# A fused attention and two-MLP kernel: order of value products, loads, one weight tile and the last product

## The reference

```python
scores = cap * tanh((q @ k.T / sqrt(64)) / cap)
attn = exp(scores - max(scores)); attn = attn / (sum(attn) + 1e-9)
x = (attn @ v), heads side by side                    # 896 x 768
x = relu(x @ w_in1) ** 2 @ w_out1                     # 768 x 2048, 2048 x 768
x = silu(x @ w_in2) @ w_out2                          # 896 x 768
```

## Time and profile before

| | |
|---|---|
| median of 3 executions | 543.65 us (543.34 to 544.69) |
| profiled execution | 543.38 us, span 541.6 us |
| TensorE (PE) busy | 530.9 us, 98% |
| VectorE (DVE) | 361.9 us, 67% |
| ScalarE (ACT) | 261.0 us, 48% |
| GpSimd (POOL) | 80.0 us, 15% |
| granted clock of TensorE | 0.998 mean |

### The profile page before, as it was taken

The page is one execution under the profiler, slowest core; times in us unless marked ns, Lnnn a source line. Parts: engine busy times, 40 slices in busy tenths (PEclk is TensorE's granted clock), DMA queues, the critical chain, the costliest instruction groups (busy, mean ns, idle before and its releaser), DMA issues.

```text
span 541.6 us, 7075 instructions
## 1 busy us (share of the span) xinstructions
PE 530.9 (98%) x2616; PEld 439.8 (81%) x2616; DVE 361.9 (67%) x623; ACT 261.0 (48%) x404; POOL 80.0 (15%) x54
## 2 busy tenths in 40 slices
PE   7999999999999999999999999999999999999996
PEld 5233334799999999999998999999999999999995
DVE  3298787687678634667789835556855345568985
ACT  5999995155443333444444344444433144454230
POOL 1899999100000000000000000000000000000000
PEclk9999999999999999999999999999999999999999
DMA  8789601051202202422022024211210241020546
GB/s 225 203 229 222 188 15 31 29 154 42 79 0 79 58 2 60 136 58 78 0 79 60 0 59 136 59 41 37 71 50 16 59 136 41 19 79 10 120 65 89
DMA packets 82117, 42.17 MB, mean 78 GB/s; under 512 B 26784, under 2 KB 79008, under 8 KB 82080
## 3 DMA queue, kind: packets, MB, share of 16 engines
q1 hardware_dynamic: 77952, 40.32, 28.9%
q10 hardware_dynamic: 4096, 1.38, 1.1%
q0 software_dynamic: 32, 0.00, 0.0%
HBM read 38.93 MB, written 2.75 MB: 77 GB/s over the span
## 4 chain that ended last, share of the span: by engine, by line
PE 81%; POOL 10%; DVE 3%; issue 2%; DMA 2%; ACT 0%; ACTq 0%; POOLq 0%; DVEq 0%
PE banks L531 26%; PE banks L532 26%; PE banks L533 26%; POOL asum L418 4%; POOL asum L415 3%; POOL asum L422 3%; PE banks L461 1%; DVE w_hl L931 1%; PE banks L454 1%; DMA qk_raw<-in_q_dram 1%; DVE y L1011 1%; DMA qk_raw<-in_k_dram 1%; PE banks L482 0%; PE banks L473 0%; ACT g_hi L733 0%
## 5 line engine op out<-in xcount | busy, mean ns | idle before, releaser
L531 PE MATMUL banks<-x_hi,w_hl 128*128 128x448 f32 x384 | 140.7, 366 | 0.0
L533 PE MATMUL banks<-x_hi,w_hl 128*128 128x448 f32 x384 | 140.5, 366 | 0.0
L532 PE MATMUL banks<-x_lo,w_hl 128*128 128x448 f32 x384 | 140.5, 366 | 0.0
L531 PE MATMUL banks<-g_hi,w_hl 128*128 128x448 f32 x336 | 123.4, 367 | 0.2 <-DVE w_hl L931 0.2
L533 PE MATMUL banks<-g_hi,w_hl 128*128 128x448 f32 x336 | 123.2, 367 | 0.0
L532 PE MATMUL banks<-g_lo,w_hl 128*128 128x448 f32 x336 | 123.2, 367 | 0.0
L531 PEld LDWEIGHTS banks<-x_hi,w_hl 128*128 128x128 f32 x384 | 72.1, 188 | 7.6 <-issue 1.4
L533 PEld LDWEIGHTS banks<-x_hi,w_hl 128*128 128x128 f32 x384 | 72.1, 188 | 6.2
L532 PEld LDWEIGHTS banks<-x_lo,w_hl 128*128 128x128 f32 x384 | 72.1, 188 | 6.2
L926 DVE TENSOR_TENSOR w_hl<-w_raw,w_hl 128x768 fp32r<-128x768 f32 x32 | 32.0, 1000 | 57.5 <-ACT w_hl L682 57.4
L714 ACT ACTIVATE work<-banks 128x448 f32<-128x448 f32 x64 | 31.3, 541 | 77.4 <-PE banks L533 68.4
(11 more groups left out here) (66 smaller groups left out, 525.7 us busy)
## 6 DMA issues: line engine op xcount, KB each, us to landing
w_raw<-in_moe_w_in_dram SPq DMA_DIRECT2D x32, 384.0 KB, 3.4
w_raw<-in_moe_w_out_dram SPq DMA_DIRECT2D x24, 512.0 KB, 5.2
qk_raw<-in_k_dram SPq DMA_DIRECT2D x44, 112.0 KB, 2.9
qk_raw<-in_q_dram SPq DMA_DIRECT2D x44, 112.0 KB, 3.3
v_t<-in_v_dram SPq DMA_DIRECT2D x24, 96.0 KB, 3.6
out_dram<-rows SPq DMA_DIRECT2D x40, 56.0 KB, 2.2
qk_raw<-in_k_dram ACTq DMA_DIRECT2D x4, 112.0 KB, 3.1
qk_raw<-in_q_dram ACTq DMA_DIRECT2D x4, 112.0 KB, 3.9
```

Of the source, the lines that this page charges most:

```text
L531: pe.matmul(dst, hi[:, kk, :], mov_hi, start=start, stop=False, skip_group_check=onto)
L532: pe.matmul(dst, hi[:, kk, :], mov_lo, start=False, stop=False, skip_group_check=onto)
L533: return pe.matmul(dst, lo[:, kk, :], mov_hi, start=False, stop=stop, skip_group_check=onto)
```

## The change

TensorE's loop makes `values(j - 1, 0)` ahead of the quarter unit of pair j; `values(j - 1, 1)` stays behind `sums`. On SyncE, part 1 of v moves from behind q and k of pair 2 to behind q and k of pair 3, and so does the quarter's v, which now stands ahead of it. On ScalarE the high part of weight tile 1 moves from behind pair 9 to behind pair 11. The last sub-product is made in two column parts, 256 and 192 columns, in two PSUM banks of their own; each part is subtracted, transposed and stored by itself, and each of the two queues issues two stores for each part. In the last group VectorE's order is changed: tile 0 is finished and transposed ahead of `prod_low(6)`.

```diff
@@ TensorE: output_first, the loops
                 pe.wait_ge(s_exp, 2 * j.n + 1)
                 values(j, 0)
-                values(j, 1)
...
             for j in range(3, PAIRS):
-                for u in range(C):
+                for u in range(CW):
                     scores(At(0, j), u)
+                output_first(At(0, j - 1))
+                scores(At(0, j), CW)
                 sums(At(0, j - 2))
-                output(At(0, j - 1))
+                values(At(0, j - 1), 1)
+                output_rest(At(0, j - 1))
@@ TensorE: model
+                if layer == 1 and s == 1 and g == GROUPS - 1 and n == NP - 1:
+                    for part, cols in enumerate(LAST_COLS):
+                        for kk in range(KQ):
+                            last = passes(last_bank(part)[:, cols], prod_split(g, n), kk,
+                                          g_hi[:, q, kk, cols], g_lo[:, q, kk, cols], kk == 0, kk == KQ - 1)
+                        last.then_inc(s_prod, 1)
+                    return
@@ common
+        LAST_T = (slice(0, 8), slice(8, QB))
+        LAST_COLS = (slice(0, 8 * BL), slice(8 * BL, S))
+        def last_bank(part):
+            return y_bank(GROUPS - 1, BANK_OF[6]) if part == 0 else y_bank(GROUPS - 2, BANK_OF[0])
@@ SyncE: loads
-                if j % 2 == 0:
+                if j % 2 == 0 and j > 2:
                     load_v(j // 2)
-                if j == 2:
+                if j == 3:
                     load_v_x()
+                    load_v(1)
@@ SyncE: stores (ScalarE likewise, with a in range(2, C))
-                for n in range(4):
+                for n in range(3 if g == GROUPS - 1 else 4):
...
+            for part, t in enumerate(LAST_T):
+                sp.wait_ge(s_rows, 4 * GROUPS + part)
+                for a in range(2):
+                    store(*y_tile(GROUPS - 1, 3), a, t)
@@ ScalarE
                 weights(At(0, j))
-                if j in (7, 9):
-                    tile_high(0, 0, (j - 7) // 2)
+                if j == 7:
+                    tile_high(0, 0, 0)
             weights(At(0, PAIRS - 1))
+            tile_high(0, 0, 1)
@@ VectorE: last group
                         post_u3(layer, s, g)
+                        if last and layer == 1 and s == 1:
+                            post_22(layer, s, g)
+                            turn_rows(g, 0, 5)
+                            prod_low(layer, s, g, 6)
+                            post_11(layer, g)
+                            turn_rows(g, 1, 6)
+                            post_21_u3(layer, g)
+                            post_12(layer, s, g)
+                            break
                         prod_low(layer, s, g, 6)
...
             leave(1, 1, GROUPS - 1, 2)
-            post_21(1, 1, GROUPS - 1)
-            leave(1, 1, GROUPS - 1, 3)
+            m, b = y_tile(GROUPS - 1, 3)
+            posted(1, 1, GROUPS - 1, 7)
+            for part, cols in enumerate(LAST_COLS):
+                dve.wait_ge(s_prod, NP * GROUPS * 2 * STAGES + part)
+                add(y[:, m, b, cols], y[:, m, b, cols], last_bank(part)[:, cols],
+                    ALU.subtract).then_inc(s_post, 1)
+                posted(1, 1, GROUPS - 1, 9 + part)
+                dve.transpose(rows[m][:, b, cols], y[:, m, b, cols]).then_inc(s_rows, 1)
```

More of the change, by code:

```diff
@@ L388, in _, with store @@
                         load_w_out(layer, s, g)
-            def store(m, b, a):
+            def store(m, b, a, t=slice(0, QB)):
                 cols = slice(m * P + BL * a, m * P + BL * a + BL)
-                sp.dma_start(out_v[b, :, :, cols],
-                             rows[m][BL * a:BL * a + BL, b, :].rearrange("p (t r) -> p t r", r=BL)
+                sp.dma_start(out_v[b, :, t, cols],
+                             rows[m][BL * a:BL * a + BL, b, :].rearrange("p (t r) -> p t r", r=BL)[:, t, :]
                              ).then_inc(s_out, DMA)
             for g in range(GROUPS):
-                for n in range(4):
+                for n in range(3 if g == GROUPS - 1 else 4):
                     m, b = y_tile(g, n)
@@ L401, in _ @@
                         store(m, b, a)
-            sp.wait_ge(s_out, DMA * B * KC * C)
+            for part, t in enumerate(LAST_T):
+                sp.wait_ge(s_rows, 4 * GROUPS + part)
+                for a in range(2):
+                    store(*y_tile(GROUPS - 1, 3), a, t)
+            sp.wait_ge(s_out, DMA * (B * KC * C + C))
         @block.gpsimd
@@ L501, in output @@
                 output_first(j)
+                values(j, 1)
                 output_rest(j)
@@ L515, in _ @@
                 output_first(At(0, j))
+                values(At(0, j), 1)
                 for u in range(1, CW):
@@ L807, in _, with store @@
                             x_high(g, 1)
-            def store(m, b, a):
+            def store(m, b, a, t=slice(0, QB)):
                 cols = slice(m * P + BL * a, m * P + BL * a + BL)
-                act.dma_start(out_v[b, :, :, cols],
-                              rows[m][BL * a:BL * a + BL, b, :].rearrange("p (t r) -> p t r", r=BL)
+                act.dma_start(out_v[b, :, t, cols],
+                              rows[m][BL * a:BL * a + BL, b, :].rearrange("p (t r) -> p t r", r=BL)[:, t, :]
                               ).then_inc(s_out, DMA)
-            for n in range(4):
+            for n in range(3):
                 act.wait_ge(s_rows, 4 * (GROUPS - 1) + n + 1)
@@ L818, in _ @@
                     store(*y_tile(GROUPS - 1, n), a)
+            for part, t in enumerate(LAST_T):
+                act.wait_ge(s_rows, 4 * GROUPS + part)
+                for a in range(2, C):
+                    store(*y_tile(GROUPS - 1, 3), a, t)
         @block.vector
@@ L1073, in x_low, with turn_rows @@
                                   ALU.subtract).then_inc(s_x, 1)
-            def turn_rows(g, n):
+            def turn_rows(g, n, after):
                 m, b = y_tile(g, n)
-                posted(1, 1, g, (5, 7, 8, 9)[n])
+                posted(1, 1, g, after)
                 dve.transpose(rows[m][:, b, :], y[:, m, b, :]).then_inc(s_rows, 1)
@@ L1085, in leave @@
                     else:
-                        turn_rows(g, n)
+                        turn_rows(g, n, (5, 7, 8, 9)[n])
             second = At(0, 1)
@@ L1200, in _ @@
                             w_s3(layer, s, g + 1)
-                        if last and layer == 1 and s == 1:
-                            leave(layer, s, g, 1)
                         if g == 1:
```

## The result

The changed kernel takes 545.07 us (median of 20 executions) beside 543.53 us for the kernel before (20 executions too): a ratio of 1.0032, with a 95% interval from 1.0024 to 1.004, that is 1.3 to 2.2 us more. The profiled execution took 544.06 us with a span of 542.3 (before: 543.38 and 541.6).

What follows compares the result with a forecast made beforehand. GpSimd was taken to set the pace of most of attention, with TensorE level. Attention +1.24, weight tile +0.3 and tail -0.2 gave +1.3 us, 544.7 for the profiled execution and 545.0 us predicted, range 543.3 to 546.2.

Steps and rivals of the forecast that it cites:

- the bound of 0.3%: What a measurement can tell from no change, 1.6 us; chances 0.35 slower, 0.62 between, 0.03 faster.
- The wait for `x_lo`: Attention: value unit 0 waits for VectorE, 2.05 us in iteration 3, 0.48 in 4, 6, 8, 10; +1.24 us, chance 0.65.
- The early load: Pair 3's q and k ahead of `v_x`: a 0.77 us wait goes, scores start sooner, nothing gained; cost nothing.
- The collision at tile 0: First hidden product: the tile's low part, arriving later, waits for a GpSimd addition; +0.3 us, bounds 0 and 0.7.
- The high part of tile 1: Moved on ScalarE from between pairs 9 and 10 to after pair 11: nothing lost, nothing won.
- The last product in two parts: Twelve matmuls of 256 and twelve of 192 columns take 2.60 to 2.81 us for 2.42; 0.3 more taken.
- the rival of slow loads: Weight loads decide the last product: over 0.122 us the parts don't pay, at 0.202 cost 2.4 us more; chance 0.08.
- The stores: Kernel's end: last store starts at 538.5, then 2.9 us to the end at 541.4; VectorE's new order eases the queues.
- The tail as a whole: Last product, its stores and VectorE's order together: -0.2 us, bounds -0.6 and +2.4.
- GpSimd keeps the pace: Attention: the wait for `x_lo` isn't met and attention ends as now; 542.8 to 543.5 us, chance 0.2.
- the change does what its parts say: Attention: waits of 0.77 and twice 0.46 us saved, no new wait, GpSimd still holds TensorE; 542.8 us, no separate chance.
- late `v_x`: Iteration 3: landing after 22.8 shifts pair 0's ones product; two us late gives 547, chance 0.04.

Runs made afterwards that it cites:

- unit_behind_quarter: Changed kernel with value unit 0 placed behind the quarter unit, ahead of the ones product; 542.21 us, ratio 0.9979 to the kernel before.
- odd_only: Changed kernel with TensorE's new order only in iterations 5, 7, 9 and 11; 542.42 us, ratio 0.9987 to the kernel before.
- order_only: Kernel before with only TensorE's new order (value unit 0 ahead of the quarter unit); 546.2 us, ratio 1.0054.
- parts_only: Kernel before with the last product in two column parts and their stores, VectorE's old order; 543.96 us, ratio 1.0008.
- dve_order_only: Kernel before with only VectorE's new order in the last group, last product in one part; 543.51 us, ratio 1.0005.
- no_order: Changed kernel with TensorE's old order put back, the other parts kept; 542.68 us, ratio 0.9987 to the kernel before.
- low_later2: Changed kernel with TensorE's old order and weight tile 0's low part moved behind the reciprocal of pair 9; 541.48 us, ratio 0.9967 to the kernel before.
- changed_again: The changed kernel executed once more, unedited; 545.08 us, ratio 1.0033 to the kernel before.
- low_early: Changed kernel with weight tile 0's low part made ahead of the sums of pair 9 on VectorE; 545.27 us, ratio 1.0039 to the kernel before.

## Why the prediction was right

**The time and the sign.** 545.0 us was forecast and 545.07 measured. The ratio, 1.0032, lies just past the bound of 0.3%, on the side to which I gave 0.35; "within 0.3%" had 0.62. The forecast was 1.3 us over the kernel before, measured are 1.74. Most of the agreement of the two times is luck. Term by term, +1.24, +0.3 and -0.2 were forecast and +1.12, +0.90 and -0.61 measured: the tile's error of +0.6 and the tail's of -0.4 nearly cancel.

**The wait for `x_lo`** was right in place, cause and size. The stand in iteration 3 was put at 2.05 us and is 1.94; the four later ones at 0.48, with 0.38 to 0.39 recorded as idle. The length of iteration 4 is the better check: 7.76 forecast (7.28 + 0.48), 7.73 measured (41.73 - 34.00). The ones product of pair 10 was forecast for 90.16 and starts at 90.29; against the kernel before, +1.24 forecast and +1.12 counted from G. `unit_behind_quarter` and `odd_only` show the cause by taking it away.

**The early load** brought forward only the scores, as said, but it was not worth nothing: beside the new order it saves the 0.18 us by which VectorE takes the first sums sooner (`order_only`). `v_x` is issued from 15.85, where 15.8 was forecast, and its last transfer lands at 21.7 (forecast: 22.2 at the latest) for a first use at 23.06. In no run with the new loads did a matmul wait for it.

**The collision at tile 0** was right in mechanism and too small in size: +0.3 was taken, and the wait is 0.87 us. The step that failed was the choice of the middle. To compare the places, 0.25 has to be taken off the changed kernel's times, since G is at 12.34 there and at 12.09 in the kernel before. GpSimd's addition was assumed to begin between 88.3 and 88.9, and it began at 88.87 (89.12), at the late end, since GpSimd had been held by late exponentials. I had written that GpSimd would have gaps, and had not carried them into its start. The low part ended at 91.78 (92.03), at the late bound of 91.8. The wait is 0.17 longer than the bound of 0.7 all the same, because TensorE was ready for the hidden product at 90.97 (91.22) and not at 91.13.

**The high part of tile 1** was costed at nothing. With the old order that holds. Beside the new one the wait at the tile is 1.24 us with the high part in its old place (`order_only`) and 0.87 in the changed kernel. The rows of `order_only` say why: the high part stands ahead of pair 10's exponentials on ScalarE, GpSimd waits 0.52 us for them at 85.47, where it doesn't wait in the changed kernel, and its first addition for pair 11 then begins only at 90.07, 0.12 us before the low part asks (0.49 in the changed kernel). No run moved the high part alone beside the new order, so that it is worth these 0.37 us is read from rows and not shown by an edit.

**The last product in two parts.** TensorE: 0.119 us per 256-column matmul ((536.45 - 535.02) / 12), forecast 0.122; 0.110 per 192-column one ((537.66 - 536.45) / 11), forecast 0.095 to 0.1125. The product takes 2.75 us for 2.42, +0.33 where I took 0.3. The shorter ones sit near the spacing of the earlier trace rows (0.1125), so the rival of slow loads falls. The Trainium skill ("TensorE: Matmul & The Clock Gate", section "LDWEIGHTS (loading the stationary operand)") prices a weight load at its columns / 1.2 ns, by estimate 107 ns for 128 columns. That lies 3 ns under these 110, and the trace agrees.

**The stores.** The tail as a whole was forecast at -0.2 and is -0.61, just past its bound. Two steps failed, in part against each other. One is the sentence that VectorE's new order eases the queues and changes nothing: I had the column parts' stores back to back on SyncE's queue and priced the order by itself. But the last store is ScalarE's. Without the new order it is issued from 539.84, 5.34 us after the last product's first matmul, and with it from 539.79, 4.77 us after, where I had 4.76 (538.5 - 533.74). The other step is the rest, from there to the end of the span: 2.9 was counted, with 0.4 for the smaller pieces, and 2.47 is measured (3.27 in the kernel before, so 0.8 less). `parts_only` and `dve_order_only` together show that each change is worth nothing or less alone, and that the gain is their product.

**The rivals.** That GpSimd keeps the pace is refuted by the chain and by the idle times in its timeline. (That it had no gap before isn't quite so: one of 0.49 us stands at 56.33 in the kernel before, in a period of 7.20.) It is what the kernel does once the order is put back (`no_order`, 542.68 us, where 542.8 to 543.5 was named for this rival). That the change does what its parts say falls with the waits of 1.94 and 0.39 us, and late `v_x` with its landing at 21.7.

## What to carry to other kernels

Before moving a product ahead in a hand-written order, look up the condition on the bank it writes: the move takes that wait forward with it, and here it cost more than the two waits it removed. Where a VectorE step with two SBUF inputs meets GpSimd's additions, its place among them mattered more than its length: put it so that it asks during the last addition that someone waits for, and the loss falls on the next. Splitting the last product paid here only once the store queues had room for the extra issues at that moment, so look at the time from the last rows' readiness to their issue.

## What the runs showed of the hardware

**The port's turn.** A VectorE subtraction that has been waiting goes ahead of GpSimd's next addition, even where GpSimd would have gone on without a gap: in `low_later2` it asked at 87.91, GpSimd's addition ended at 88.85, and the low part ended at 89.67, as GpSimd's next addition grew by 0.6 us.

**A spacing that changes by itself.** Long stretches of identical matmuls of 448 columns run at one of three spacings, 202.7, 204.0 or 206.7 ns (means over a hundred matmuls and more), under a granted clock of 1.00. The windows view gives length, busy time with the count of matmuls, and granted clock, here for 165 to 195 us of the kernel before and of the changed one:

```profile
165.00:195.00 30.00, 30.00 (x147) 1.00 0.22 62
```

```profile
165.00:195.00 30.00, 30.00 (x150) 1.00 0.22 62
```

Three matmuls more in the same 30 us, on a stretch that the change doesn't touch, are 0.6 us; over the whole stretch (162 to 202 us) it is about 1 us between the two profiles, in favour of the changed kernel. That is why the two spans differ by 0.7 us where the books give 1.4 and G lies 0.25 later. Which spacing a stretch takes varied between kernels, and `changed_again` had that of the changed kernel. From the first hidden product to the last product it made 442.5 to 444.4 us over the fourteen profiles, so a single span can't show a gain of 1 us; the timed ratios of the changed kernel, `order_only` and `dve_order_only` follow the books (+1.7, +2.9 and +0.3 us, for +1.4, +2.6 and +0.1) and not this length; that of `low_early` lies above both (+2.1, for +0.9). What sets the spacing was not tried and stays open.
